# A three-stage attention and expert kernel: x parts in three joined pieces, and a rearranged hand-over

## The chip, the cores and the metric

The kernel runs on one core of a Trainium2 chip. The metric is the device time of one execution in microseconds, from the median of several runs. Engines: TensorE (PE, and PEld for its weight loads), VectorE (DVE), ScalarE (ACT), GpSimd (POOL), SyncE (SP), which issues the loads.

## The reference, cut to what matters

```
attn_out = attention(q, k, v)              # window 128 and 4 sink keys; 2 x 8 heads x 768 x 64
x = attn_out as 1536 rows of 512
assign each row to one of 8 experts, 192 rows each
for e in range(8):                          # w1[e] 512 x 1024, w2[e] 1024 x 512
    x[mask] = relu(x[mask] @ w1[e]) @ w2[e]
return ((x @ w_a) * (x @ w_b)) @ w_out      # 512 x 1536 twice, 1536 x 512
```

## The kernel before, in words

**Precision.** Every fp32 operand is kept as a high part, rounded to fp32r by a copy on ScalarE, and a low part, the difference, made on VectorE or GpSimd. A product is high x high, high x low and low x high.

**Experts.** After attention and routing, `expert(e)` runs eight times. An expert has four weight units u = 0 to 3 (two halves of w1, two of w2), each 128 x 2048. SyncE loads a unit to `raw[u]`, ScalarE rounds it in two halves (`split_hi`, L790), the low parts go to `ring_lo[u]`: for u = 0 to 2 on VectorE in halves (`split_lo`, L1012), for u = 3 on GpSimd in one instruction (L625). Each unit gives two groups g = 0, 1: ScalarE copies a part of the sum from PSUM (L936), VectorE adds (L1401 or L1404), and for u < 2 ScalarE and VectorE write the high and low part of h (L943, L1418). Unit u = 2, 3 of TensorE waits for `w_lo[u]`.

**Mixing stages.** The last product is done in two halves of the rows (c = 0, 1), each in six stages, so n = 0 to 11. Each half of 768 rows is two blocks of HT = 384. A stage has `mix(0, n)` (a factor of w_a), `down(n - 1)` (times w_out) and `mix(1, n)` (w_b). `mix` uses seven products P1, P6, P2, P7, P5, P4, P3 in that order instead of eight, with four sums of weight blocks (`add_blocks`, L688 to L695, GpSimd) and four sums T1 to T4 of blocks of x (`add_t`, L653 to L658, GpSimd). `round_mix(u, n, 0)` and `(u, n, 1)` on ScalarE round the plain blocks (L899, L900) and the sums (L904); `split_mix` on GpSimd makes the low parts (L704, four instructions, 1792 elements a partition); `round_out` (L913) and `split_out` (L718) do the same for w_out. `keep_p1` (L969) copies P1 from PSUM, and P2 on TensorE waits for it. `keep_a11` (L975) copies the first factor block. `round_g` (L982) and `lower_b` (L1433) split the product of the two factors for `down`.

**Parts of x.** The seven blocks of x of one half (B11, B21, B22, T1 to T4; 768 elements a partition each) are made in pieces of `PIECE` columns: `add_t(c, q)`, then `round_t(c, q)` (ScalarE, L923), then `split_t(c, q)` (GpSimd, L664). Before there are four pieces of 96 columns, with 7 instructions of 128 x 192 for each rounding and each low part. For c = 0 they stand in experts 4, 5, 6 and a fourth at the end of expert 6; for c = 1 the sums stand in stages n = 1 to 4, rounding and low parts in stages 2 to 5.

**What sets the order.** Each engine's list is written out by hand and runs in order; an instruction that waits for a semaphore holds up all behind it. In the last expert ScalarE's list has `round_mix(0,0,0)` after group (2,0), `round_mix(0,0,1)` after (2,1), `round_mix(1,0,0)` after (3,0), and `round_mix(1,0,1)` and `round_out(0)` behind the expert. GpSimd's list there is `split_lo(7, 3)` and then `add_blocks(0, 0)`, which waits for it, since the weight sums `s_sum` lie in `raw[3]`.

Of the kernel before, what the change touches and what calls it, by code (L numbers as in the profile page):

```python
# [5 lines left out]
def attention_moe_gated_product_kernel(  # L6
# [12 lines left out]
    f32 = mybir.dt.float32  # L19
# [37 lines left out]
    PIECE = HT // 4  # L57
# [16 lines left out]
    with ctx:  # L74
# [107 lines left out]
        t_tmp = sb("t_tmp", [P, 4, 2, PIECE])  # L182
# [211 lines left out]
        T4, T1, T2, T3, B11, B21, B22 = range(7)  # L394
# [17 lines left out]
        s_sum = raw[3][:, 0:4 * 2 * P].rearrange("p (b t m) -> p b t m", b=4, t=2)  # L412
        p1_sb = raw[2][:, 2 * DM:2 * DM + HT]
        u2_sb = raw[2][:, 2 * DM + HT:2 * DM + 2 * HT]
        u3_sb = raw[3][:, 4 * 2 * P:4 * 2 * P + HT]
# [16 lines left out]
        def t_block(c, b, low):  # L432

            if c == 0:
                return two(x_block(0, b) if low else t_first[:, b, :])
            if not low:
                return two(x_block(1, b))
            if b < 4:
                return two((ring[3], ring_lo[3])[b // 2][:, b % 2 * 2 * HT:(b % 2 + 1) * 2 * HT])
            return t_last[:] if b == B22 else two(x_block(b - B11, 7))  # L440

        def t_sources(c, q):

            first, second = (y[c][:, :, h * HT + q * PIECE:h * HT + (q + 1) * PIECE] for h in range(2))
            return {B11: first[:, 0:2, :], B21: first[:, 2:4, :], "B12": second[:, 0:2, :], B22: second[:, 2:4, :],
                    T4: t_tmp[:, T4], T1: t_tmp[:, T1], T2: t_tmp[:, T2], T3: t_tmp[:, T3]}

        def t_moves(c, q, low):

            qs = slice(q * PIECE, (q + 1) * PIECE)  # L450
            return [(b, t_block(c, b, low)[:, :, qs]) for b in (B11, B21, B22, T4, T1, T2, T3)]
# [114 lines left out]
        def _(pool):  # L566
# [78 lines left out]
            def add_t(c, q):  # L645

                src = t_sources(c, q)
                k = 4 * c + q
                if q == 0:
                    pool.wait_ge(grp_done, 8 * 4 * (c + 1))  # L650
                if k > 0:
                    pool.wait_ge(t_split, k)
                nc.gpsimd.tensor_tensor(src[T1], src["B12"], src[B11], ALU.subtract).then_inc(t_sums, 1)  # L653
                nc.gpsimd.tensor_tensor(src[T3], src[B22], src["B12"], ALU.subtract).then_inc(t_sums, 1)
                pool.wait_ge(t_sums, 4 * k + 1)
                nc.gpsimd.tensor_tensor(src[T2], src[B22], src[T1], ALU.subtract).then_inc(t_sums, 1)
                pool.wait_ge(t_sums, 4 * k + 3)
                nc.gpsimd.tensor_tensor(src[T4], src[B21], src[T2], ALU.subtract).then_inc(t_sums, 1)  # L658

            def split_t(c, q):  # L660
                src = t_sources(c, q)
                pool.wait_ge(t_rounded, 4 * c + q + 1)
                for (b, lo), (_, hi) in zip(t_moves(c, q, 1), t_moves(c, q, 0)):
                    op = nc.gpsimd.tensor_tensor(lo, src[b], hi.bitcast(f32), ALU.subtract)  # L664
                op.then_inc(t_split, 1)
# [3 lines left out]
            for e in range(4, E):  # L669
                if e < E - 1:  # L670
                    add_t(0, e - 4)
                split_lo(e, 3)
                if e < E - 1:
                    split_t(0, e - 4)
                if e == E - 2:
                    add_t(0, 3)
                    split_t(0, 3)
            def add_blocks(u, n):
# [5 lines left out]
                if k == 0:  # L684
                    pool.wait_ge(*expert_split(E - 1, 3))
                else:
                    pool.wait_ge(unit_lo[1 - u], n + u)
# [43 lines left out]
            for n in range(STAGES):  # L731
# [5 lines left out]
                if 2 <= n <= 5:  # L737
                    split_t(1, n - 2)
# [7 lines left out]
                if 1 <= n <= 4:  # L746
                    add_t(1, n - 1)
# [34 lines left out]
        def _(act):  # L782
# [132 lines left out]
            def round_t(c, q):  # L915

                src = t_sources(c, q)
                k = 4 * c + q
                if q == 0:
                    act.wait_ge(grp_done, 8 * 4 * (c + 1))  # L920
                act.wait_ge(t_sums, 4 * (k + 1))
                for b, dst in t_moves(c, q, 0):
                    op = nc.scalar.activation(dst, src[b], ACT.Copy)  # L923
                op.then_inc(t_rounded, 1)

            def expert(e, first):
                last = e == E - 1
                for u in range(4):
# [3 lines left out]
                    for g in range(2):  # L932
# [16 lines left out]
                        if e == E - 2 and (u, g) == (3, 1):  # L949
                            round_t(0, 3)  # L950
                        if last and (u, g) == (2, 0):
                            round_mix(0, 0, 0)
                        if last and (u, g) == (2, 1):
                            round_mix(0, 0, 1)
                        if last and (u, g) == (3, 0):
                            round_mix(1, 0, 0)
# [3 lines left out]
            round_mix(1, 0, 1)  # L960
            round_out(0)

# [21 lines left out]
            for n in range(STAGES):  # L984
# [7 lines left out]
                if 2 <= n <= 5:  # L992
# [15 lines left out]
        def _(dve):  # L1008
# [385 lines left out]
            def expert(e, first):  # L1394
                for u in range(4):
                    for s, bk in (EARLY_TILES[0] if u == 0 and first else late_tiles(e, u)):
                        split_x(s, bk)
                    for g in range(2):
# [21 lines left out]
                        if more and urgent:  # L1420
                            split_lo(e + 1, half // 2, half % 2)

# [33 lines left out]
            def factor_b(n):  # L1456
# [21 lines left out]
                lower_b(n, 1)  # L1478
                dve.wait_ge(products_b, 7 * n + P3)
# [3 lines left out]
                lower_b(n, 2)  # L1483
# [22 lines left out]
        def _(pe):  # L1506
# [301 lines left out]
            def mix(u, n):  # L1808
# [4 lines left out]
                if u == 0:  # L1813
                    if n % PAIRS_F == 0:
                        pe.wait_ge(t_split, 4 * (c + 1))
# [80 lines left out]
```

## Time and profile before

| what | us |
|---|---|
| median of 3 runs | 670.22 (668.29 to 672.74) |
| the profiled execution | 673.89 |
| its span | 672.1 |
| TensorE busy | 612.9 (91%) |
| VectorE / ScalarE / GpSimd busy | 402.1 / 320.4 / 329.8 |
| last experts' end, mixing stages | about 380; 382 to 666 |

The chain that ended last goes by TensorE for 68% of the span and by GpSimd for 16%. Matmul spans are modelled and overlap, so a stretch where TensorE is busy all the time is read against its neighbours, not as peak.

### The profile page before, as it was taken

The numbers are of one execution on the slowest core, as the hardware profiler recorded it, in microseconds if no ns is written. First come the engines' busy times: TensorE is split into PE (matmuls) and PEld (weight loads), VectorE is DVE, ScalarE is ACT, GpSimd is POOL, SyncE is SP. The second block draws the span as 40 slices with busy tenths as digits, with TensorE's granted clock in tenths as the row PEclk, the third lists the DMA queues.
The fourth block names the chain that finished last, engine by engine and source line by source line (L and its number), as shares of the span: only waits on it lengthen the run. The fifth ranks groups of instructions, "written<-read, shape, count | busy, mean of one in ns | idle before, by whom it ended". The sixth has DMA issues, their size and how long they took to land.

```text
span 672.1 us, 10960 instructions
## 1 busy us (share of the span) xinstructions
PE 612.9 (91%) x3840; PEld 548.3 (82%) x3840; DVE 402.1 (60%) x1060; ACT 320.4 (48%) x804; POOL 329.8 (49%) x371
## 2 busy tenths in 40 slices
PE   7999999999543999999997799999999999999995
PEld 4877766776322899999997799998999989999983
DVE  4567755764674377766874145665566466556654
ACT  3577656753231376767776333452453334344310
POOL 4000000000003321235787997999999888777623
PEclk8798999989655899999999889999999999999999
DMA  9974142130402456567565122221122242211002
GB/s 187 262 149 94 49 132 65 28 123 25 149 0 62 129 189 208 187 233 238 198 212 183 47 67 90 64 64 62 64 66 91 64 151 70 95 32 32 31 1 94
DMA packets 87512, 72.07 MB, mean 107 GB/s; under 512 B 39840, under 2 KB 74656, under 8 KB 87456
## 3 DMA queue, kind: packets, MB, share of 16 engines
q1 hardware_dynamic: 85536, 65.05, 33.1%
q0 software_dynamic: 1920, 6.29, 2.8%
q8 instruction: 32, 0.52, 0.3%
q14 instruction: 24, 0.20, 0.1%
HBM read 65.04 MB, written 6.29 MB: 106 GB/s over the span
## 4 chain that ended last, share of the span: by engine, by line
PE 68%; POOL 16%; DVE 7%; ACT 5%; issue 3%; DMA 1%; DVEq 0%; POOLq 0%; ACTq 0%
PE psum L1760 12%; PE psum L1838 6%; PE psum L1840 6%; PE psum L1841 6%; PE psum L1573 6%; PE psum L1761 6%; POOL w_lo L704 5%; PE psum L1753 3%; PE psum L1755 3%; PE psum L1754 3%; PE psum L1551 3%; PE psum L1538 3%; PE psum L1578 2%; PE psum L1515 2%; POOL x_hl L664 2%
## 5 line engine op out<-in xcount | busy, mean ns | idle before, releaser
L704 POOL TENSOR_TENSOR w_lo<-w_raw,w_hi 128x512 fp32r<-128x512 f32 x96 | 107.8, 1160 | 19.0 <-ACT w_hi L900 19.0
L1760 PE MATMUL psum<-h_hl,w_hi 128*128 128x384 f32 x256 | 77.3, 370 | 3.9 <-DVE h_hl L1418 3.8
L629 POOL MEMSET thr<- 128x8 f32 x1 | 0.1, 106 | 163.4 <-PE psum L1658 163.4
L1760 PE MATMUL psum<-x_hl,w_hi 128*128 128x384 f32 x256 | 76.8, 370 | 1.8 <-DVE x_hl L1387 1.6
L1840 PE MATMUL psum<-x_hl,w_hi 128*128 128x384 f32 x216 | 72.8, 337 | 0.0
L790 ACT ACTIVATE w_hi<-w_raw 128x1024 fp32r<-128x1024 f32 (+1 forms) x72 | 69.0, 958 | 0.0
L1494 DVE TENSOR_TENSOR o_acc<-psum,o_acc 128x512 f32<-128x512 f32 x60 | 41.5, 692 | 42.1 <-PE psum L1755 42.1
L1761 PE MATMUL psum<-x_hl,w_lo 128*128 128x192 f32 x256 | 65.0, 254 | 0.0
L1761 PE MATMUL psum<-h_hl,w_lo 128*128 128x192 f32 x256 | 65.0, 254 | 0.0
L1838 PE MATMUL psum<-t_first,w_hi 128*128 128x384 f32 x168 | 57.4, 341 | 6.4 <-ACT w_raw L969 4.1
L1753 PE MATMUL psum<-o_hi,g 128*128 128x512 f32 x144 | 56.1, 389 | 2.3 <-issue 2.3
L625 POOL TENSOR_TENSOR w_lo<-w_raw,w_hi 128x2048 fp32r<-128x2048 f32 x7 | 32.3, 4609 | 52.2 <-ACT w_hi L790 52.2
L1838 PE MATMUL psum<-x_hl,w_hi 128*128 128x384 f32 x168 | 56.3, 335 | 0.6 <-DVE w_raw L1447 0.6
L1841 PE MATMUL psum<-t_first,w_lo 128*128 128x384 f32 x168 | 56.7, 337 | 0.0
L1755 PE MATMUL psum<-o_hi,g 128*128 128x512 f32 x144 | 56.3, 391 | 0.0
L1754 PE MATMUL psum<-o_lo,g 128*128 128x512 f32 x144 | 56.2, 390 | 0.0
L1841 PE MATMUL psum<-x_hl,w_lo 128*128 128x384 f32 x168 | 56.2, 335 | 0.0
L1012 DVE TENSOR_TENSOR w_lo<-w_raw,w_hi 128x1024 fp32r<-128x1024 f32 x42 | 55.8, 1330 | 0.0
L904 ACT ACTIVATE w_hi<-w_raw 128x512 fp32r<-128x512 f32 x48 | 27.6, 624 | 53.6 <-POOL w_raw L695 53.6
L810 ACT ACTIVATE p_sb<-psum,nmax 128x264 f32<-128x264 f32 (+1 forms) x96 | 43.3, 459 | 20.3 <-DVE nmax L1038 20.3
L1760 PEld LDWEIGHTS psum<-h_hl,w_hi 128*128 128x128 f32 x256 | 49.0, 192 | 4.5 <-DVE w_lo L1012 3.3
L982 ACT ACTIVATE g<-psum 128x384 fp32r<-128x384 f32 x48 | 23.6, 492 | 60.9 <-DVE psum L1473 26.3
(220 smaller groups left out, 1606.3 us busy)
## 6 DMA issues: line engine op xcount, KB each, us to landing
w_raw<-in_moe_w_dram SPq DMA_DIRECT2D x32, 1024.0 KB, 5.5
w_raw<-in_moe_w_a_dram SPq DMA_DIRECT2D x12, 512.0 KB, 3.6
w_raw<-in_moe_w_b_dram SPq DMA_DIRECT2D x12, 512.0 KB, 3.5
w_raw<-in_moe_w_out_dram SPq DMA_DIRECT2D x12, 512.0 KB
k_raw<-in_k_dram SPq DMA_DIRECT2D x16, 192.0 KB, 3.8
q_raw<-in_q_dram SPq DMA_DIRECT2D x16, 192.0 KB, 4.1
v_sb<-in_v_dram SPq DMA_DIRECT2D x16, 192.0 KB, 4.2
xs_scratch<-x_rows SPq DMA_DIRECT2D x8, 384.0 KB, 3.4
```

Source lines behind the costliest of these rows:

```text
L704: return nc.gpsimd.tensor_tensor(out_t, t, hi_t.bitcast(f32), ALU.subtract)
L790: op = nc.scalar.activation(ring[slot][:, ps], raw[r][:, ps], ACT.Copy)
L810: op = nc.scalar.activation(p_sb[:, t % 2, h * SW:(h + 1) * SW][:, span(t, h)], bank[2 * (t % 2) + h][:, span(t, h)], ACT.Exp, scale=-1.0, ...
L1012: op = nc.vector.tensor_tensor(ring_lo[slot][:, hs], raw[slot][:, hs], ring[slot][:, hs].bitcast(f32), ALU.subtract)
L1753: nc.tensor.matmul(o, lhs_hi, rhs_hi, start=first, stop=False)
L1754: nc.tensor.matmul(o, lhs_hi, rhs_lo, start=False, stop=False)
L1755: return nc.tensor.matmul(o, lhs_lo, rhs_hi, start=False, stop=final)
L1760: nc.tensor.matmul(bk[:, 0:2 * CAP], lhs_hi, rhs_both, start=first, stop=False)
L1761: return nc.tensor.matmul(bk[:, 0:CAP], lhs_lo, rhs_hi, start=False, stop=final)
L1838: nc.tensor.matmul(o, w_h, t_hi[:, t, :], start=(first and t == 0), stop=False, skip_group_check=True)
L1840: nc.tensor.matmul(o, w_h, t_lo[:, t, :], start=False, stop=False, skip_group_check=True)
L1841: last = nc.tensor.matmul(o, w_l, t_hi[:, t, :], start=False, stop=(t == 1), skip_group_check=True)
```

## The change

The parts of x come in three pieces of 128 columns. Blocks that lie side by side are rounded and lowered together: 4 instructions of 512, 512, 512 and 256 elements a partition for a piece. T3 is written over the block B12 in y, so it waits for T1. The block order is changed to make this possible. Pieces of c = 0 stand in experts 4, 5 and 6; those of c = 1 have their sums in stages 1 to 3 and the rest in stages 2 to 4. `s_sum` moves to `raw[2]` beside the w_out unit, and the copies p1, u2, u3 to `raw[3]`. The last expert's unit 3 low parts are made by VectorE in two halves, after groups (1,1) and (2,0). ScalarE's first four `round_mix` come one group sooner, and `round_out(0)` comes after `keep_a11(0)`. In the last stage `lower_b` of part 2 comes before the P3 sum.

```diff
-    PIECE = HT // 4
+    PIECES = 3
+    PIECE = HT // PIECES
...
-        t_tmp = sb("t_tmp", [P, 4, 2, PIECE])
+        t_tmp = sb("t_tmp", [P, 3, 2, PIECE])
...
-        T4, T1, T2, T3, B11, B21, B22 = range(7)
+        T4, T1, T3, B22, B11, B21, T2 = range(7)
...
-        s_sum = raw[3][:, 0:4 * 2 * P].rearrange("p (b t m) -> p b t m", b=4, t=2)
-        p1_sb = raw[2][:, 2 * DM:2 * DM + HT]
-        u2_sb = raw[2][:, 2 * DM + HT:2 * DM + 2 * HT]
-        u3_sb = raw[3][:, 4 * 2 * P:4 * 2 * P + HT]
+        s_sum = raw[2][:, 2 * DM:2 * DM + 4 * 2 * P].rearrange("p (b t m) -> p b t m", b=4, t=2)
+        p1_sb, u2_sb, u3_sb = (raw[3][:, at * HT:(at + 1) * HT] for at in range(3))
...
-                    T4: t_tmp[:, T4], T1: t_tmp[:, T1], T2: t_tmp[:, T2], T3: t_tmp[:, T3]}
-
-        def t_moves(c, q, low):
-
-            qs = slice(q * PIECE, (q + 1) * PIECE)
-            return [(b, t_block(c, b, low)[:, :, qs]) for b in (B11, B21, B22, T4, T1, T2, T3)]
+                    T4: t_tmp[:, 0], T1: t_tmp[:, 1], T2: t_tmp[:, 2], T3: second[:, 0:2, :]}
+
+        def blocks_at(t, q):
+
+            return t.rearrange("p (m n) -> p m n", n=HT)[:, :, q * PIECE:(q + 1) * PIECE]
+
+        def t_moves(c, q):
+
+            first, second = (y[c][:, :, h * HT + q * PIECE:h * HT + (q + 1) * PIECE] for h in range(2))
+            x_c = x_hl[:, :, c * N:(c + 1) * N]
+            in_x = [blocks_at(x_c[:, t, :], q) for t in range(3)] + [blocks_at(x_c[:, 3, 0:2 * HT], q)]
+            sources = (t_tmp[:, 0:2].rearrange("p b t n -> p (b t) n"), second, first, t_tmp[:, 2])
+            if c == 0:
+                flat = t_first[:].rearrange("p b n -> p (b n)")
+                hi = [blocks_at(flat[:, t * 4 * HT:min((t + 1) * 4, 14) * HT], q) for t in range(4)]
+                return list(zip(hi, in_x, sources))
+            ends = x_hl[:, 3, :].rearrange("p (c z m n) -> p c z m n", c=2, z=2, n=HT)[:, :, 1, :,
+                                                                                       q * PIECE:(q + 1) * PIECE]
+            lo = [blocks_at(ring[3][:, 0:4 * HT], q), blocks_at(ring_lo[3][:, 0:4 * HT], q), ends,
+                  t_last[:, :, q * PIECE:(q + 1) * PIECE]]
+            moves = list(zip(in_x, lo, sources))
+            moves[2] = (*(t.rearrange("p (u m) n -> p u m n", u=2) if t is not ends else t for t in moves[2]),)
+            return moves
...
                 nc.gpsimd.tensor_tensor(src[T1], src["B12"], src[B11], ALU.subtract).then_inc(t_sums, 1)
+                pool.wait_ge(t_sums, 4 * k + 1)
                 nc.gpsimd.tensor_tensor(src[T3], src[B22], src["B12"], ALU.subtract).then_inc(t_sums, 1)
-                pool.wait_ge(t_sums, 4 * k + 1)
                 nc.gpsimd.tensor_tensor(src[T2], src[B22], src[T1], ALU.subtract).then_inc(t_sums, 1)
...
-            for e in range(4, E):
-                if e < E - 1:
-                    add_t(0, e - 4)
+            for e in range(4, E - 1):
+                add_t(0, e - 4)
                 split_lo(e, 3)
-                if e < E - 1:
-                    split_t(0, e - 4)
-                if e == E - 2:
-                    add_t(0, 3)
-                    split_t(0, 3)
+                split_t(0, e - 4)
...
                 if k == 0:
-                    pool.wait_ge(*expert_split(E - 1, 3))
+                    pool.wait_ge(*expert_split(E - 1, 2))
...
-                if 2 <= n <= 5:
+                if 2 <= n < 2 + PIECES:
                     split_t(1, n - 2)
...
-                if 1 <= n <= 4:
+                if 1 <= n < 1 + PIECES:
                     add_t(1, n - 1)
...
                         if 4 <= e < E - 1 and (u, g) == (2, 1):
                             round_t(0, e - 4)
-                        if e == E - 2 and (u, g) == (3, 1):
-                            round_t(0, 3)
+                        if last and (u, g) == (1, 1):
+                            round_mix(0, 0, 0)
                         if last and (u, g) == (2, 0):
-                            round_mix(0, 0, 0)
+                            round_mix(0, 0, 1)
                         if last and (u, g) == (2, 1):
-                            round_mix(0, 0, 1)
+                            round_mix(1, 0, 0)
                         if last and (u, g) == (3, 0):
-                            round_mix(1, 0, 0)
+                            round_mix(1, 0, 1)
 
             for e in range(E):
                 expert(e, e == 0)
-            round_mix(1, 0, 1)
-            round_out(0)
...
                 if n > 0:
                     round_mix(1, n, 1)
-                if 2 <= n <= 5:
+                else:
+                    round_out(0)
+                if 2 <= n < 2 + PIECES:
                     round_t(1, n - 2)
...
                             split_lo(e + 1, half // 2, half % 2)
+                        if e == E - 1 and (u, g) in ((1, 1), (2, 0)):
+                            split_lo(e, 3, u - 1)
...
                 lower_b(n, 1)
+                if n == STAGES - 1:
+                    lower_b(n, 2)
                 dve.wait_ge(products_b, 7 * n + P3)
...
-                lower_b(n, 2)
+                if n < STAGES - 1:
+                    lower_b(n, 2)
```

## Rows read from the trace of the kernel before

**Rows 1.** TensorE by windows: stretch, length, busy (x) of each engine, granted clock, DMA

```profile
365.00:370.00 5.00, 1.22 (x8) 0.99 (x8) 3.85 (x6) 4.08 (x8) 4.74 (x7) 1.00 0.24 79
387.80:390.60 2.80, 2.80 (x9) 2.80 (x10) 0.56 (x1) 0.49 (x1) 2.80 (x3) 0.50 0.01 3
```

**Rows 2.** TensorE's waits from 340 us on: total, times, longest

```profile
PE psum L1838 <- ACT w_raw L969: 4.1, 3, 3.2
```

**Rows 3.** ScalarE in order of time: start, duration, idle before and releaser in brackets

```profile
363.30 0.87 ACT L923 ACTIVATE t_first<-y 128x192 fp32r<-128x192 f32 x3 [5.64 <-POOL t_tmp L658]
...
385.26 1.15 ACT L904 ACTIVATE w_hi<-w_raw 128x512 fp32r<-128x512 f32 x2 [4.43 <-POOL w_raw L695]
386.31 1.04 ACT L913 ACTIVATE o_hi<-w_raw 128x1024 fp32r<-128x1024 f32 x1
387.26 0.47 ACT L969 ACTIVATE w_raw<-psum 128x384 f32<-128x384 f32 x1
```

**Rows 4.** GpSimd in order of time: low parts of unit (0,0)

```profile
377.71 4.45 POOL L704 TENSOR_TENSOR w_lo<-w_raw,w_hi 128x512 fp32r<-128x512 f32 x4
```

**Rows 5.** ScalarE: copies of group (2,0) in experts 5 and 6

```profile
332.01 0.33 ACT L936 ACTIVATE grp_sb<-psum 128x192 f32<-128x192 f32 x1 [1.50 <-PE psum L1761]
...
350.57 0.33 ACT L936 ACTIVATE grp_sb<-psum 128x192 f32<-128x192 f32 x1 [1.50 <-PE psum L1761]
```

**Rows 6.** GpSimd in experts 5 and 6: an x piece, one instruction of it, unit 3

```profile
317.75 2.70 POOL L664 TENSOR_TENSOR x_hl<-y,t_first 128x192 fp32r<-128x192 f32 x3 [6.85 <-ACT t_first L923]
318.86 1.59 POOL L664 TENSOR_TENSOR x_hl<-y,t_first 128x192 fp32r<-128x192 f32 x1
320.41 4.24 POOL L664 TENSOR_TENSOR x_hl<-t_tmp,t_first 128x192 fp32r<-128x192 f32 x4
...
345.64 4.63 POOL L625 TENSOR_TENSOR w_lo<-w_raw,w_hi 128x2048 fp32r<-128x2048 f32 x1
```

**Rows 7.** VectorE beside the blocked instruction

```profile
318.73 1.25 DVE L1012 TENSOR_TENSOR w_lo<-w_raw,w_hi 128x1024 fp32r<-128x1024 f32 x1
```

**Rows 8.** Three stages by windows, from down product to down product

```profile
431.76:454.54 22.78, 22.78 (x121) 21.34 (x121) 13.61 (x24) 10.24 (x23) 22.55 (x30) 1.00 0.23 70
454.54:477.74 23.20, 23.07 (x122) 21.31 (x121) 13.61 (x24) 10.10 (x23) 22.97 (x29) 1.00 0.21 69
477.74:501.27 23.53, 23.08 (x121) 21.32 (x121) 13.61 (x24) 10.15 (x24) 23.29 (x30) 1.00 0.22 68
```

**Rows 9.** GpSimd in these stages, in order of time

```profile
427.79 4.50 POOL L704 TENSOR_TENSOR w_lo<-w_raw,w_hi 128x512 fp32r<-128x512 f32 x4 [1.42 <-ACT w_hi L900]
...
438.36 0.73 POOL L695 TENSOR_TENSOR w_raw<-w_raw 128x256 f32<-128x256 f32 x1
...
461.84 0.74 POOL L695 TENSOR_TENSOR w_raw<-w_raw 128x256 f32<-128x256 f32 x1
...
469.47 0.61 POOL L653 TENSOR_TENSOR t_tmp<-y 128x192 f32<-128x192 f32 x1
...
471.84 0.74 POOL L688 TENSOR_TENSOR w_raw<-w_raw 128x256 f32<-128x256 f32 x1
...
474.76 4.51 POOL L704 TENSOR_TENSOR w_lo<-w_raw,w_hi 128x512 fp32r<-128x512 f32 x4
479.23 1.16 POOL L664 TENSOR_TENSOR x_hl<-y,x_hl 128x192 fp32r<-128x192 f32 x2
...
483.14 0.75 POOL L688 TENSOR_TENSOR w_raw<-w_raw 128x256 f32<-128x256 f32 x1
...
485.36 0.73 POOL L695 TENSOR_TENSOR w_raw<-w_raw 128x256 f32<-128x256 f32 x1
```

**Rows 10.** ScalarE in the last stage: part 2 of the factor product

```profile
655.47 0.49 ACT L982 ACTIVATE g<-psum 128x384 fp32r<-128x384 f32 x1 [0.57 <-DVE psum L1477]
```

**Rows 11.** VectorE in the last stage: low parts 2 and 3

```profile
656.88 1.21 DVE L1433 TENSOR_TENSOR g<-psum,g 128x384 fp32r<-128x384 f32 x2
```

More of the change, by code:

```diff
@@ L439, in t_block @@
                 return two((ring[3], ring_lo[3])[b // 2][:, b % 2 * 2 * HT:(b % 2 + 1) * 2 * HT])
-            return t_last[:] if b == B22 else two(x_block(b - B11, 7))
+            return t_last[:] if b == T2 else two(x_block(b - B11, 7))
         def t_sources(c, q):
@@ L647, in add_t @@
                 src = t_sources(c, q)
-                k = 4 * c + q
+                k = PIECES * c + q
                 if q == 0:
@@ L660, in split_t @@
             def split_t(c, q):
[L661 to L664, printed above, removed]
+                pool.wait_ge(t_rounded, PIECES * c + q + 1)
+                for hi, lo, src in t_moves(c, q):
+                    op = nc.gpsimd.tensor_tensor(lo, src, hi.bitcast(f32), ALU.subtract)
                 op.then_inc(t_split, 1)
@@ L915, in round_t @@
             def round_t(c, q):
-                src = t_sources(c, q)
-                k = 4 * c + q
+                k = PIECES * c + q
                 if q == 0:
@@ L921, in round_t @@
                 act.wait_ge(t_sums, 4 * (k + 1))
-                for b, dst in t_moves(c, q, 0):
-                    op = nc.scalar.activation(dst, src[b], ACT.Copy)
+                for hi, _, src in t_moves(c, q):
+                    op = nc.scalar.activation(hi, src, ACT.Copy)
                 op.then_inc(t_rounded, 1)
@@ L1814, in mix @@
                     if n % PAIRS_F == 0:
-                        pe.wait_ge(t_split, 4 * (c + 1))
+                        pe.wait_ge(t_split, PIECES * (c + 1))
                     if n == 0:
```

## The prediction, made before the change was run

> **What bounds the kernel now.** I read the stages by windows, then TensorE's waits, then the other engines in order of time. From the fourth w_out stage on, the mixing stages are TensorE's own: a plain one lasts 22.78 us and TensorE is busy for all of it, [rows 8], first line. The kernel loses time in two places, and both belong to the queues that feed TensorE.
>
> The first is the hand-over from the last expert to the first mixing unit. Of the 5 us after 365.0 TensorE works 1.22 [rows 1], and later it waits up to 3.2 us in one piece for ScalarE's L969 [rows 2]. Two causes stand in a row. ScalarE's second x round in expert 6 (fourth quarter) stood 5.64 us behind GpSimd's sums [rows 3], with expert 7's first group copy queued behind it. Then GpSimd's low parts of unit (0,0) ended at 377.71 + 4.45 = 382.16 [rows 4], its sums for unit (1,0) were ready for ScalarE at 385.26, and the kept P1 (L969), which TensorE's third product waits for, was queued behind that rounding and behind the w_out rounding: 387.26, so TensorE went on half a microsecond later, at 387.8, where the second window of [rows 1] begins (the sum takes 387.78). After these 3.2 us without work the granted clock was 0.50 for 2.80 us, the 1.2 GHz level: half of that, 1.40, is lost.
>
> The second is the mixing stages in which GpSimd also makes the parts of x for the second half. Call D the start of a stage's down product (the window's start) and L the start of L695, the last weight sum of unit (0, n+1). L - D is 6.60, 7.30 and 7.62 in the first three windows and these last 22.78, 23.20 and 23.53 [rows 8, 9]: a stage is long by L - D - 6.87 where that is positive. One more stage is like the third (+0.73), so the excess is 0.42 + 0.75 + 0.73 = 1.90 us. Between two L695 lie 23.5 us in which GpSimd never waits.
>
> **Hand-over.** The fourth quarter of x is gone from expert 6: no second x round, no second GpSimd turn. Expert 7 then follows in the rhythm of the group copies, 350.57 - 332.01 = 18.56 us [rows 5]: its group (2,0) is copied at 350.57 + 18.56 = 369.13.
> - Unit (0,0)'s first copy is now issued behind group (1,1), some 2 us ahead of this, and its sums are made by GpSimd right after the x piece, near 364, since GpSimd's own low parts of unit 3 (4.6 us, [rows 6]) are gone from in front of them; both are early. ScalarE's groups (2,0) to (3,1) get one rounding each queued ahead of them, and only the last, the (3,1) copy, is late by it (below). SyncE's loads of the first units and of w_out wait for the same low parts as before, which come earlier; they cost nothing. The roundings of the sums follow the (2,0) copy: 369.4 to 370.5 (1.15 for the two, [rows 3]).
> - VectorE makes both low halves of unit 3. The second comes after group (2,0): 369.85 to 371.1 (1.25, [rows 7]). TensorE could begin unit 3 some 0.5 behind the group, at 369.65, and waits until 371.3, then runs a quarter of the rhythm, 4.64, to 375.95. That stall of 1.6 is hidden by the chain below and too short for the clock, as far as these rows go.
> - A GpSimd instruction that starts inside such a VectorE instruction stands until it ends: one at 318.86 took 1.59 us where its three took 2.70 together, so the other two 0.56 each [rows 6, 7]. So GpSimd's third low part starts not at 370.6 but at 371.15, and the last two (2.5 of the 4.45, [rows 4]) end at 373.65.
> - From there as before: 382.16 to 385.26 is 3.10, the two roundings 1.05 (385.26 to 386.31), no w_out rounding (it moved behind the kept A11) but one group copy (0.33 long, [rows 5], of which some 0.1 overlaps, as 1.15 and 1.05 show), and 0.52 from L969 to TensorE [rows 3]. 373.65 + 3.10 + 1.05 + 0.25 + 0.52 = 378.57.
> - A product has 6 x 384 columns; a plain stage has 50,688 columns in 22.78 us [rows 8], so a product takes 1.04. TensorE has done two of unit (0,0) by 378.05 and idles 0.5.
>
> 387.78 - 378.57 = 9.21 gained, plus 1.40 of half clock that no long gap now causes. The w_out rounding then runs 380.05 to 381.1, GpSimd's w_out low parts 381.2 to 383.7, sums and low parts of unit (0,1) to 391.2, where TensorE wants them twelve products on, at 378.57 + 12.48 = 391.05; I charge 0.2. **Hand-over: -10.4 us.** Bounds: -12.8 if everything ran end to end from 365.04 (two expert units 9.28, two products 2.08: third product at 376.4, and 1.4 of clock); -3.8 if only the idle time of the first window went. Each step has its row, so I keep the computed value.
>
> The Trainium skill ("GPSIMD Engine Reference", section 8, Key points) says that GpSimd shares its SBUF interfaces with VectorE and contends with instructions that have two SBUF inputs. This speaks against moving the low parts to VectorE, which puts two such instructions beside GpSimd's low parts. If the whole of both (2 x 1.25) were lost to GpSimd instead of the 0.55 that I charge, the hand-over would give 8.4, the rival A below; the 1.59 us row agrees with the rule for starts inside, but a wide GpSimd instruction under two of them took 4.63 [rows 6], so an instruction already running is not held.
>
> **Joined pieces in the experts.** Per piece ScalarE and GpSimd have 4 instructions of 512, 512, 512 and 256 elements, as [rows 4]'s 4.45 us; before 7 of 192, 3.91 where nothing is in the way (479.23 to 483.14, [rows 9]) and 2.70 + 4.24 = 6.94 in expert 5, three starts blocked [rows 6]. Now also two or three starts are blocked: 4.45 + 2.1 = 6.5. The sums grow from 2.37 (469.47 to 471.84) to 3.05: four of 256, 2.92 (471.84 to 474.76), and one more wait for the one before, 0.13. So GpSimd is some 0.2 later with unit 3's low parts, which ended at 345.64 + 4.63 = 350.27 while TensorE needs them at about 351.1 (just behind the group of 350.57, [rows 5, 6]): covered, cost 0. Without that cover each 1 us later in experts 5 and 6 costs 1 us. ScalarE's share per piece is unchanged, 1.9. The exchange of s_sum and the p1, u2, u3 buffers costs nothing: it lets the sums start on unit 2's low parts.
>
> **Joined pieces in the mixing stages.** Here nothing hides them. A piece's low parts cost 4.45 + 0.02 = 4.47 against 3.91, its sums 3.05 against 2.37, in three stages instead of four. The first sums are absorbed: GpSimd stands 1.42 us for ScalarE behind them, before 427.79 [rows 9]. First stage: L - D = 6.60 + 0.56 = 7.16, excess 0.29. Second and third: GpSimd's 23.50 becomes 23.50 - 3.91 - 2.37 + 4.47 + 3.05 = 24.74, so each exceeds 22.78 by 1.96. The fourth: 23.50 - 6.28 = 17.2, none. Total 0.29 + 1.96 + 1.96 = 4.21 against 1.90: **+2.3 us**. The same work in fewer instructions, but packed into fewer stages that were already full. Bounds: if the joined ones cost no more than the old piece, 0; at 5.2 ns an element (6.94 over 1344), the slow rows of the experts, +16.8 (rival B). The mixing rows are much the nearer.
>
> **Tail.** In the last stage part 2's lowering moves ahead of the P3 sum and product. ScalarE rounds that part at 655.47 to 655.96 [rows 10]; VectorE lowered it at 656.88 [rows 11], now at 656.0, so the down product starts 0.88 sooner. The last part comes some 0.7 later, needed by tile 3 four us on: covered. **-0.9 us.** The bound above is 0, if something else holds the down product.
>
> **Sum:** -10.4 + 2.3 - 0.9 = -9.0. The profiled execution took 673.89 (span 672.1), giving 664.9; it stands 3.67 above the median of 670.22, so the timed median would be **661.2**.
>
> **The rivals.**
> - **A, the hand-over keeps a wait.** Contention on GpSimd (-8.4 there) or a TensorE gap on unit 3's low parts that reaches 3 us and halves the clock (another 1.4). For: four queues cross here. Against: the chain is short. Sum -7.0 to -5.6: 663.2 to 664.6. Chance 0.17.
> - **B, slower.** The joined instructions of the mixing stages run at the slow rows' rate: 9.3 us a piece. Excess is 3x - 9.2 for a piece of x us, so 18.7, or +16.8 on before: -10.4 + 16.8 - 0.9 = +5.5, 675.7. It decides from x = 7.5. Against: GpSimd's like-shaped four took 4.51 in these very stages [rows 9]. Chance 0.05.
> - **C, the pieces hold up the experts.** Each of experts 5 and 6 loses about 2 us, as GpSimd's low parts of unit 3 pass TensorE's need: 661.2 + 4.4 = 665.6. For: only 0.8 us of slack. Chance 0.12.
> - **D, the hand-over is all gained** and the mixing stages pay less: -12.8 + 1 - 0.9 = -12.7, 657.5. Chance 0.09.
> - That the rearrangement does nothing, since TensorE is bound anyway: the idle windows speak against it; 669 to 671, chance 0.05.
>
> **Numbers.** Forecast 0.52. A change of 1% is 6.7 us, about what a measurement can tell, so faster means below 663.5: forecast mostly (0.47), D, and part of A (0.06): 0.62. Within 1%: the rest of forecast and A, C and the last: 0.32. Slower by over 1%: 0.06, B and accidents. The range takes in D at one end and A and C at the other, 657.0 to 667.0.
>
> **What would show it.** Hand-over: no second x round in expert 6, the gap at 365 gone, third product of unit (0,0) near 378.6 at full clock, ScalarE's L969 behind a group copy and not behind the w_out rounding. Mixing: two stages of about 24.7 us and L695 about 8.8 after D, the next one plain. Experts: groups every 18.56 us. Tail: part 2 lowered before the P3 sum, the last down product 0.9 sooner after it. Wrong if the two long stages are near 30 us, if experts 5 and 6 lose time, or if TensorE idles over 3 us before the first product.

## The result, and the profile after

The changed kernel took 661.54 us (660.15 to 662.47), beside 670.22 (668.29 to 672.74) for the kernel before on the same chip: 8.7 less, a ratio of 0.987, 95% interval 0.982 to 0.991. These and all ratios below are of fast executions; a fourth one of the kernel before, 680.88, was in the chip's slower state and is left out. Its profiled execution took 662.47 (span 660.7), 11.4 less than the one of before.

I cut both traces at the same instructions. "Third product" is that of unit (0,0) which waits for the kept P1; D1 is the first down product. The second, third and fourth row make up the hand-over, from group (2,0) of expert 6 to D1. The forecast of the first row is its value before.

| stretch | before | predicted | after |
|---|---|---|---|
| to the (2,0) copy of expert 6 | 350.57 | 350.57 | 347.91 |
| (2,0) copy, expert 6 to expert 7 | 24.33 | 18.56 | 19.30 |
| from there to the third product | 12.88 | 9.44 | 9.57 |
| from there to D1 | 21.19 | 19.99 | 20.26 |
| D1 to D6 (where the pieces of c = 1 lie) | 115.81 | 118.12 | 118.08 |
| D6 to D12 | 132.75 | 131.87 | 131.00 |
| D12 to the end | 14.57 | 14.57 | 14.58 |

(D12 is the last down product.) The hand-over gave 9.27 of the 10.4 forecast. The 2.66 ahead of it and the 0.87 between D6 and D7 are not the change's: they are absent in a repeat of the same kernel (e5). Of the 2.66, 1.35 had been gained before the first expert product (218.32 in place of 219.67), in attention.

Two lines of the page after, busy times and the chain that ended last:

```profile
PE 606.7 (92%) x3840; PEld 541.9 (82%) x3840; DVE 410.2 (62%) x1062; ACT 317.0 (48%) x772; POOL 321.4 (49%) x330
...
PE 70%; POOL 14%; DVE 6%; ACT 5%; issue 3%; DMA 1%; DVEq 0%; ACTq 0%; POOLq 0%
```

TensorE's waits from 300 us on (total, times, longest), where [rows 2] had one of 3.2:

```profile
PE psum L1852 <- ACT w_raw L976: 3.5, 3, 1.7
PE psum L1774 <- DVE w_lo L1021: 1.8, 1, 1.8
PE psum L1767 <- issue: 1.4, 1, 1.4
PE psum L1774 <- POOL w_lo L641: 1.4, 2, 0.8
```

L976 is the kept P1: 0.23 us at the third product, the rest in the two long stages. L641 is unit 3's low parts on GpSimd, 0.85 and 0.51 us in experts 5 and 6, which I had forecast as covered. ScalarE in the last expert:

```profile
367.21 0.33 ACT L946 ACTIVATE grp_sb<-psum 128x192 f32<-128x192 f32 x1 [1.56 <-PE psum L1775]
...
374.97 1.16 ACT L915 ACTIVATE w_hi<-w_raw 128x512 fp32r<-128x512 f32 x2 [0.78 <-POOL w_raw L706]
376.03 0.32 ACT L946 ACTIVATE grp_sb<-psum 128x192 f32<-128x192 f32 x1
376.24 0.48 ACT L976 ACTIVATE w_raw<-psum 128x384 f32<-128x384 f32 x1
...
378.53 1.05 ACT L924 ACTIVATE o_hi<-w_raw 128x1024 fp32r<-128x1024 f32 x1
```

This is the order that was forecast: only a group copy stands between the rounding of the sums and L976, and the w_out rounding comes behind ([rows 3] had it in front). GpSimd beside it:

```profile
365.73 2.66 POOL L715 TENSOR_TENSOR w_lo<-w_raw,w_hi 128x512 fp32r<-128x512 f32 x2 [2.45 <-ACT w_hi L911]
368.66 3.19 POOL L715 TENSOR_TENSOR w_lo<-w_raw,w_hi 128x512 fp32r<-128x512 f32 x2 [0.28 <-ACT w_hi L915]
```

The second pair, beside VectorE's low half of unit 3, takes 3.19 against 2.66: the 0.5 charged for it is there. The five stages by windows, in the columns of [rows 8]:

```profile
397.04:419.82 22.78, 22.78 (x121) 21.34 (x121) 13.61 (x24) 10.28 (x20) 19.77 (x23) 1.00 0.23 70
419.82:442.89 23.07, 23.07 (x121) 21.30 (x121) 13.61 (x24) 9.42 (x19) 22.76 (x26) 1.00 0.21 69
442.89:467.64 24.75, 23.07 (x122) 21.30 (x122) 13.61 (x24) 10.14 (x21) 24.44 (x27) 1.00 0.20 65
467.64:492.33 24.69, 23.08 (x121) 21.31 (x121) 13.61 (x24) 8.90 (x18) 23.16 (x24) 1.00 0.19 64
492.33:515.12 22.79, 22.79 (x122) 21.35 (x122) 13.60 (x24) 8.41 (x16) 17.18 (x19) 1.00 0.21 70
```

Excess over 22.78 from the second on: 0.29, 1.97, 1.91 and nothing (forecast 0.29, 1.96, 1.96, 0). In the third GpSimd is busy for 24.44 of 24.75 and TensorE for 23.07. TensorE's own waits in the two long stages, 1.6 to 1.7 each, are for L976, which ScalarE reaches only after rounding GpSimd's sums. That GpSimd's load sets the length is tested by e1. Its last weight sums:

```profile
426.99 0.74 POOL L706 TENSOR_TENSOR w_raw<-w_raw 128x256 f32<-128x256 f32 x1
...
451.74 0.75 POOL L706 TENSOR_TENSOR w_raw<-w_raw 128x256 f32<-128x256 f32 x1
...
476.43 0.73 POOL L706 TENSOR_TENSOR w_raw<-w_raw 128x256 f32<-128x256 f32 x1
```

L - D is 7.17, 8.85 and 8.79 (forecast 7.16 for the first; 8.83 would follow from 1.96 + 6.87).

### The profile page after: what moved, and what is told of

It reads as the page before. It is cut to its first block, busy times and chain, and to the rows that moved or that the text cites. A ratio compares the mean times of both kernels' runs of the same rounds, so it can differ in the third digit from the quotient of the medians.

```text
span 660.7 us, 10889 instructions
## 1 busy us (share of the span) xinstructions
PE 606.7 (92%) x3840; PEld 541.9 (82%) x3840; DVE 410.2 (62%) x1062; ACT 317.0 (48%) x772; POOL 321.4 (49%) x330
## 4 chain that ended last, share of the span: by engine, by line
PE 70%; POOL 14%; DVE 6%; ACT 5%; issue 3%; DMA 1%; DVEq 0%; ACTq 0%; POOLq 0%
PE psum L1774 13%; PE psum L1852 6%; PE psum L1855 6%; PE psum L1854 6%; PE psum L1775 6%; PE psum L1587 6%; POOL w_lo L715 5%; PE psum L1767 4%; PE psum L1769 4%; PE psum L1768 4%; PE psum L1565 3%; PE psum L1552 3%; PE psum L1592 2%; PE psum L1529 2%; POOL x_hl L679 2%
## 5 line engine op out<-in xcount | busy, mean ns | idle before, releaser
L715 POOL TENSOR_TENSOR w_lo<-w_raw,w_hi 128x512 fp32r<-128x512 f32 x96 | 109.3, 1174 | 21.6 <-ACT w_hi L911 21.2
L1774 PE MATMUL psum<-h_hl,w_hi 128*128 128x384 f32 x256 | 75.4, 363 | 3.1 <-DVE w_lo L1021 1.8
L1774 PE MATMUL psum<-x_hl,w_hi 128*128 128x384 f32 x256 | 75.5, 366 | 1.6 <-DVE x_hl L1396 1.6
L1775 PE MATMUL psum<-x_hl,w_lo 128*128 128x192 f32 x256 | 64.8, 253 | 0.0
L1021 DVE TENSOR_TENSOR w_lo<-w_raw,w_hi 128x1024 fp32r<-128x1024 f32 x44 | 64.8, 1472 | 0.0
L1775 PE MATMUL psum<-h_hl,w_lo 128*128 128x192 f32 x256 | 64.2, 251 | 0.0
L641 POOL TENSOR_TENSOR w_lo<-w_raw,w_hi 128x2048 fp32r<-128x2048 f32 x6 | 27.7, 4610 | 50.7 <-ACT w_hi L801 50.7
L1774 PEld LDWEIGHTS psum<-h_hl,w_hi 128*128 128x128 f32 x256 | 48.0, 188 | 3.8 <-DVE w_lo L1021 2.0
```

The source lines that it names most:

```text
L715: return nc.gpsimd.tensor_tensor(out_t, t, hi_t.bitcast(f32), ALU.subtract)
L1021: op = nc.vector.tensor_tensor(ring_lo[slot][:, hs], raw[slot][:, hs], ring[slot][:, hs].bitcast(f32), ALU.subtract)
L1774: nc.tensor.matmul(bk[:, 0:2 * CAP], lhs_hi, rhs_both, start=first, stop=False)
L1775: return nc.tensor.matmul(bk[:, 0:CAP], lhs_lo, rhs_hi, start=False, stop=final)
```

## The experiments

Ratios are to the kernel before on the same chip, with 95% intervals. Unless it is said otherwise a kernel is the changed one with the edit shown, and nothing is left out of the computation. Where an edit is long, the fence tells it in words. The interval of every ratio overlaps that of the changed kernel (0.982 to 0.991; those of e1 and e11 only at its lower edge), so what a part is worth is read from the traces, not from the times. "Rhythm" is the distance between the same group copies of two experts, and "hand-over" is the sum of the three rows named above (before 58.40, changed 49.13). "Chain" is the distance from expert 7's (2,0) copy to the third product (changed: 9.57). "F to E" is from the first expert product to the end of the span (before 452.4, changed 442.4, the changed kernel again 446.6); it leaves out attention, which no kernel here touches.

**e1: the second half in four joined pieces.** It separates packing from the joining itself.

```diff
-    PIECES = 3
+    PIECES = (3, 4)          # by half; FIRST = (0, 3)
```

> The changed kernel, but the parts of x of the second half (c = 1) in four joined pieces of 96 columns, in stages 1 to 5 as before the change; the first half keeps three pieces. My theory (a mixing stage is long by L - D - 6.87, L the start of the last weight sum, D the start of the down product): a piece's low parts cost 3.5 us and its sums 2.45, so GpSimd's period falls from 24.7 to 23.2; L - D about 6.2, 6.6, 7.05, 7.3; excess 0, 0, 0.2, 0.4 instead of 0.3, 2.0, 1.9: 3.6 us faster than the changed kernel, near 658. Rival: what makes the two stages long is ScalarE's joined rounding or the new buffers, not GpSimd's load; then the excess stays about 4 us, only spread over more stages.

Ratio 0.978 (0.973 to 0.983). The stages:

```profile
422.29:445.08 22.79, 22.79 (x122) 21.34 (x121) 13.60 (x24) 9.97 (x20) 22.48 (x27) 1.00 0.21 70
445.08:467.87 22.79, 22.79 (x122) 21.35 (x122) 13.60 (x24) 9.99 (x20) 22.48 (x26) 1.00 0.23 71
467.87:490.72 22.85, 22.85 (x122) 21.30 (x121) 13.60 (x24) 9.84 (x20) 22.53 (x27) 1.00 0.21 70
490.72:513.90 23.18, 23.08 (x121) 21.32 (x121) 13.60 (x24) 8.23 (x16) 21.67 (x24) 1.00 0.21 69
```

The excess is 0.45 in place of 4.17 (and of 1.90 before). Joining is a gain; packing four pieces into three turned it into a loss. F to E is 442.6, 4.0 below the changed kernel in the same rhythm (e5), where 3.6 were expected. Against the changed kernel's first profile, 442.4, nothing shows, since that one had the shorter rhythm.

**e5: the changed kernel again.** Not an edit: it tells the change from the execution.

> The changed kernel once more, beside the others of this call. All theories: the stages as in its first trace (22.8, 23.1, 24.7, 24.7, 22.8); in the experts a rhythm of 18.56 us like the five others, not the 18.21 of its first trace, so 2 to 3 us above its first 661.5.

Ratio 0.987 (0.983 to 0.991), hand-over 49.29, stages 23.06, 24.70, 24.68 and again a plain one. But the expert rhythm was 18.56 as before, where the first profile of the same kernel had 18.21, and D6 to D7 was 23.72. The rhythm was expected; the median, 665.28 on another chip, is 3.7 above the first one's where 2 to 3 were. The hand-over is made up differently: 18.48 + 10.67 + 20.14. The chain is 1.1 longer because TensorE's 1.8 us wait was followed by half clock here:

```profile
371.00:374.00 3.00, 2.44 (x9) 2.44 (x10) 0.77 (x2) 0.65 (x2) 2.88 (x2) 0.63 0.00 0
374.00:377.00 3.00, 3.00 (x19) 3.00 (x19) 0.00 (x0) 0.00 (x0) 2.90 (x5) 0.80 0.58 174
```

and in the first profile of the same kernel it was not:

```profile
369.40:372.00 2.60, 2.48 (x17) 2.48 (x18) 0.33 (x2) 0.23 (x1) 2.46 (x3) 1.00 0.00 0
```

The number behind the five busy times is the granted clock: 0.63 and 0.80 against 1.00. In the matmuls of e5 one sees the 1.2 GHz level and its end:

```profile
371.56 0.53 PE L1774 MATMUL psum<-h_hl,w_hi 128*128 128x384 f32 x1 [1.79 <-DVE w_lo L1021]
...
374.72 0.57 PE L1774 MATMUL psum<-h_hl,w_hi 128*128 128x384 f32 x1
...
375.51 0.36 PE L1774 MATMUL psum<-h_hl,w_hi 128*128 128x384 f32 x1
```

Two products later the third starts at 379.91, with no wait for ScalarE left: TensorE had become the later of the two.

**e2: unit 3's low parts of the last expert on GpSimd again.**

```diff
+            split_lo(E - 1, 3)           # GpSimd, behind the experts' pieces
...
-                        if e == E - 1 and (u, g) in ((1, 1), (2, 0)):
-                            split_lo(e, 3, u - 1)
```

> The changed kernel, but the last expert's unit 3 low parts on GpSimd again, in one instruction ahead of the first weight sums. My theory: the instruction fits into GpSimd's idle time there (3.7 us before the first low parts of unit (0,0)), and VectorE no longer holds it up, so the third product of unit (0,0) starts within 0.7 us of the changed kernel's and the 1.8 us wait of TensorE for unit 3 goes; total within 1 us of the changed kernel. Rival: moving these low parts off GpSimd is what pays in the hand-over, and 3 to 4.6 us come back.

Ratio 0.987 (0.980 to 0.994), hand-over 49.21. The 1.8 us wait is gone, and the third product waits 2.48 instead (chain 10.05). The clock stays at 1.00 behind the 2.48. The chain lies between the changed kernel's 9.57 and its 10.67 with half clock (e5), so the move to VectorE gains 0.5 or loses 0.6: it trades one wait for another. In e2 the weight sums again wait for unit 3's low parts on GpSimd, so what the new place of `s_sum` gives the hand-over is undone here too.

**e3: ScalarE's order as before.**

```diff
-   round_mix after groups (1,1), (2,0), (2,1), (3,0); round_out after keep_a11(0)
+   round_mix after groups (2,0), (2,1), (3,0), behind the expert; then round_out(0)
```

> The changed kernel, but ScalarE's first four roundings of weights one group later, as before the change, and the w_out rounding and the second rounding of unit (1,0) ahead of the kept P1. My theory: the low parts of unit (0,0) end 1 us later and the kept P1 another 1 us later behind the w_out rounding, so 1.5 to 2 us slower than the changed kernel, with no half clock. Rival: the order carries most of the hand-over: 5 us or more come back, with a gap over 3 us and the half clock.

Ratio 0.990 (0.987 to 0.993), hand-over 51.43. The w_out rounding stands in front of the kept P1 (L977 here):

```profile
377.18 1.04 ACT L924 ACTIVATE o_hi<-w_raw 128x1024 fp32r<-128x1024 f32 x1
378.13 0.47 ACT L977 ACTIVATE w_raw<-psum 128x384 f32<-128x384 f32 x1
```

The third product waits 3.01, the chain is 11.82 (2.25 more), and then the clock falls:

```profile
378.65:382.00 3.35, 3.35 (x12) 3.35 (x13) 0.56 (x1) 0.49 (x1) 3.35 (x4) 0.58 0.08 20
```

From the third product to D1 it took 21.16, 0.9 more than with the changed order. The order is worth 2.25 + 0.9 against the changed kernel's first profile, and 1.15 + 1.0 against e5, which has the half clock itself; expected were 1.5 to 2 and no half clock.

**e4: the first half in four joined pieces, the fourth at the end of expert 6.**

```diff
-    PIECES = 3
+    PIECES = (4, 3)
...
+            add_t(0, 3)                  # GpSimd, behind the experts
+            split_t(0, 3)
...
+                        if e == E - 2 and (u, g) == (3, 1):
+                            round_t(0, 3)
```

> The changed kernel, but the parts of x of the first half in four joined pieces of 96 columns, the fourth at the end of expert 6 as before the change; the second half keeps three. My theory: ScalarE stands for GpSimd's sums at the end of expert 6 with expert 7's first group copy behind it, TensorE idles near 365, and 3 to 5 us of the hand-over gain are lost. Rival: the low parts moved to VectorE and the new order are what pays, and this costs under 1 us, since the joined quarter is short.

Ratio 0.994 (0.990 to 0.997), hand-over 52.72: 23.29 + 9.19 + 20.24. The step from expert 6 to 7 is long again, for the reason of [rows 3]:

```profile
361.95 0.53 ACT L939 ACTIVATE t_first<-t_tmp 128x384 fp32r<-128x384 f32 x1 [5.04 <-POOL t_tmp L678]
```

TensorE waits 2.04 and 0.70 us for it, and the 3.2 us behind them ran at a granted clock of 0.50. Pieces of 96 columns leave unit 3 of experts 5 and 6 without a wait: the rhythm into expert 6 is 18.56, where the changed kernel has 19.30.

**e6: unit 3's low parts ahead of the sums of x** in experts 4 to 6, against the 0.85 and 0.51.

```diff
             for e in range(4, E - 1):
-                add_t(0, e - 4)
                 split_lo(e, 3)
+                add_t(0, e - 4)
```

> The changed kernel, but GpSimd makes unit 3's low parts ahead of the sums of x in experts 4 to 6. My theory: TensorE's two waits for them (0.5 to 0.85 each, the rival C of the prediction in small) go, the sums still come in time for ScalarE's rounding, 1.3 us faster than the changed kernel. Rival: TensorE's time in the experts is set by VectorE, which the long GpSimd instructions hold up; then the waits only move to VectorE's low parts and nothing is gained.

Ratio 0.988 (0.985 to 0.991), hand-over 50.71. My theory fell. The waits for GpSimd are gone, but ScalarE now stands for the sums, its copies come late, and TensorE waits for h instead (the second row is a sum of two, the longer 0.7):

```profile
PE psum L1774 <- DVE w_lo L1021: 2.0, 1, 2.0
PE psum L1774 <- DVE h_hl L1427: 1.1, 2, 0.7
```

The steps between experts became 19.36 and 19.72, in an execution with the 18.21 rhythm; e7, with the same order in the other rhythm, has 18.56 and 19.26, together as much as e5's 19.31 and 18.48. Nothing is gained in either.

**e9: the first half's blocks one by one,** seven instructions of 256 elements a piece instead of four joined.

```diff
-                return list(zip(hi, in_x, sources))
+                return [each of the moves, cut into blocks of 2 x 128 columns]
```

> The changed kernel, but in experts 4 to 6 each joined copy and each joined low part is split into blocks of 256 elements (seven for a piece on each engine); the second half stays joined. My theory: the long GpSimd instructions hold VectorE's low parts of the weights (1.8 to 2.3 us instead of 1.2 to 1.6), and with short ones these go back under 1.7; but GpSimd itself is held at more starts, so the low parts of unit 3 come no earlier and TensorE's waits in experts 5 and 6 stay or grow to 1 us each: total equal to the changed kernel within 2 us. Rival: length is the harm, and with short ones both waits go, 1 us faster.

Ratio 0.989 (0.985 to 0.993). TensorE waits 1.5 and 0.8 for unit 3's low parts, the steps are 19.99 and 19.23, and the x piece takes 7.9 us against 7.4. VectorE is relieved (1.49 where the joined piece makes it 2.04; its three low parts beside the piece take 4.08 together, against 5.45 in the changed kernel and 4.25 before), while GpSimd takes longer:

```profile
315.36 1.49 DVE L1026 TENSOR_TENSOR w_lo<-w_raw,w_hi 128x1024 fp32r<-128x1024 f32 x1
```

**e10: the tail's order as before** (one execution).

```diff
-                if n == STAGES - 1:
-                    lower_b(n, 2)
```

> The changed kernel, but in the last stage part 2 is lowered behind the P3 sum and product, as before the change. My theory: the last down product starts 0.88 us later (its distance from the one before 17.95 us, not 17.07), the rest of the trace as before; the single time says nothing at this size. Rival: the last down product waits for something else, and its distance stays.

665.41 in one execution. The last down product comes 17.95 us after the one before, against 17.07; its wait is

```profile
PE psum L1764 <- issue: 2.3, 1, 2.3
```

against 1.4: 0.88, exactly the forecast term. The hand-over of this trace is 18.45 + 9.56 + 20.26.

**e7, e8, e11: combinations.** All have e1's pieces and the order of e11's first two edits below. e7 and e8 add e6's order, and e8 also e2's placement. e11 puts VectorE's halves of unit 3 sooner:

```diff
-                            round_mix(1, 0, 1)     # after group (3,0)
+   round_mix(1, 0, 1) behind keep_p1 of unit (0,0)
-   split_out(0) ahead of unit (0,1)'s low parts
+   split_out(0) behind them
-                        if e == E - 1 and (u, g) in ((1, 1), (2, 0)):
-                            split_lo(e, 3, u - 1)
+                        if e == E - 1 and u == 1:
+                            split_lo(e, 3, g)
```

> The changed kernel with the second half of x in four joined pieces, unit 3's low parts ahead of the sums in experts 4 to 6, unit (1,0)'s sums rounded behind the kept P1, and w_out's first low parts behind those of unit (0,1). My theory adds up: -3.6 (stages), -1.3 (experts), -0.5 to -2.5 (hand-over, since no chain by the kept P1 is left and TensorE's own work sets it): 5.5 to 7.5 us faster than the changed kernel of this call. Rival: the hand-over is bound by GpSimd's low parts whatever the order; then 4.9.

658.55 us, 0.981 (0.976 to 0.985); hand-over 48.26, F to E 441.1.

> As the one before, but the last expert's unit 3 low parts on GpSimd in one instruction. My theory: TensorE's 1.8 us wait for unit 3 goes, but GpSimd's low parts of unit (0,0) come 2 us later and set the first product; within 1 us of the one before. Rival: VectorE's part matters once the kept P1 no longer waits: 2 us slower.

660.83 us, 0.982 (0.980 to 0.984); hand-over 48.55, F to E 440.8. As the theory had it, the wait for unit 3 is gone and TensorE waits 1.19 for GpSimd's low parts of unit (0,0) instead. The median is 2.3 above e7's, as the rival had it, but F to E is 0.3 below e7's: the difference lies ahead of the experts and is not the edit's.

> The changed kernel with the second half in four joined pieces, unit (1,0)'s sums rounded behind the kept P1, w_out's first low parts behind those of unit (0,1), and VectorE's two halves of unit 3 in the last expert after groups (1,0) and (1,1) instead of (1,1) and (2,0); the order of the low parts in experts 4 to 6 as in the changed kernel. My theory: TensorE's wait of 1.8 to 2.0 us for unit 3, behind which the clock was at half in three of five traces, goes; 1 to 2 us faster than the best of the last call (658.5), near 657. Rival: GpSimd's low parts of unit (0,0), now under VectorE's, come later and TensorE waits for them instead: no gain.

659.51 us, 0.979 (0.975 to 0.983); hand-over 45.61 (18.50 + 7.03 + 20.08), F to E 439.0. TensorE has no wait between expert 7 and the stages:

```profile
368.00:371.00 3.00, 3.00 (x23) 2.97 (x22) 1.96 (x4) 2.33 (x7) 2.46 (x2) 1.00 0.00 0
371.00:374.00 3.00, 3.00 (x24) 3.00 (x23) 0.12 (x1) 0.86 (x3) 2.86 (x4) 1.00 0.00 0
```

F to E is the smallest of all, 7.6 below e5 in the same rhythm. In the timed runs the intervals of e1, e7 and e11 overlap, so that e11 is faster than e1 is shown by the traces alone; the 657 that was expected was missed. All three have central values of 0.981 or less (the changed one: 0.987, twice), but none is clear of the changed kernel's interval.

## Why the prediction was right

It was right in the mechanisms that carry the sum and nearly right in the sum; two of its claims failed, "covered, cost 0" and "too short for the clock". The terms are these.

**The sum.** The terms found give -9.27 + 2.27 - 0.88 = -7.9, and expert 5 loses 0.75 ahead of the hand-over (e5): -7.1 against a forecast of -9.0. The profiles give -11.4 (the first) and -7.5 (e5, span 664.6), the medians -8.7 and, on e5's chip, -8.4. From F to E they are -10.0 and only -5.8: the first has the shorter rhythm and lacks the 0.87 at D6 to D7, and e5 loses 1.1 in its first experts, before the first piece of x. The interval of e5's ratio (0.983 to 0.991, that is 6 to 12 us) holds all of these but the -5.8. So the forecast was somewhat too large by its own terms, and the timed runs can't tell the two apart. That the median came within 0.4 of the 661.2 forecast is in part luck.

**Hand-over, -10.4 forecast, -9.3 found.** Part by part: expert 6 to 7, -5.77 forecast and -5.03 found; the chain, -3.44 and -3.31; the third product to D1, -1.20 and -0.93. The working of the chain, 9.44, was right to 0.13: low parts slowed by 0.5, roundings, group copy, L976. The 5.77 holds more than the idle windows that the prediction names: in the kernel before there was a second stretch of half clock, in expert 7, from 370.30 to 373.54 at a granted clock of 0.50, behind waits of 3.06 and 0.72 us. It went with them. What failed is named next. By experiments: without the fourth quarter the step from expert 6 to 7 is 4.0 to 4.8 shorter (23.29 in e4, 18.45 to 19.30 without); ScalarE's order is worth 2.25 of the chain and 0.9 behind it (e3); the halves on VectorE next to nothing (e2). In e3 and e4 the total moves by less than the part (2.2 and 3.5), because what is undone in one part lets another run better: e4's chain is 9.19. The two were not undone together, so of the 9.2 some 3.5 is given to no part by an experiment.

**The failed step: "covered, cost 0"** for the pieces in the experts. I gave a piece 6.5 us and GpSimd a slack of 0.8. The piece takes 7.4, from 314.79 to 320.50 + 1.72 = 322.22:

```profile
314.79 1.29 POOL L679 TENSOR_TENSOR x_hl<-t_tmp,t_first 128x512 fp32r<-128x512 f32 x1 [6.29 <-ACT t_first L933]
316.04 4.50 POOL L679 TENSOR_TENSOR x_hl<-y,t_first 128x512 fp32r<-128x512 f32 x2
320.50 1.72 POOL L679 TENSOR_TENSOR x_hl<-t_tmp,t_first 128x256 fp32r<-128x256 f32 x1
325.34 4.59 POOL L641 TENSOR_TENSOR w_lo<-w_raw,w_hi 128x2048 fp32r<-128x2048 f32 x1
```

Unit 3's low parts end at 329.93, and TensorE goes on at 329.99 after 0.85 of waiting. From the (2,0) copy of the expert before they end 19.53 later, against 18.26 in the kernel before: GpSimd is 1.3 later, not 0.2, which is 0.5 more than the slack of 0.8. In the rhythm of 18.56 TensorE indeed waits 0.5 (e5), and in that of 18.21, which leaves less slack, 0.85.

Such a wait lengthens the step by 0.24 more than itself: 0.75 with a wait of 0.51 (e5, 18.56 to 19.31), 1.09 with 0.85 (first profile, 18.21 to 19.30). The first profile's second step is 19.30 too, but with a wait of only 0.51. The other 0.34 is TensorE's own. It starts a pair of products (L1774 and L1775) every 284.5 ns up to the wait, 62 pairs from 330.36 to 348.00, and every 290.0 ns behind it, 62 from 349.32 to 367.30, at a granted clock of 1.00. In e5 it goes the other way, 290.0 from 332.88 to 350.86 and 284.5 from 351.69 to 369.33, and this is why its second step is as short as 18.48. So the two steps came to 0.6 to 0.8 more than two plain ones (e1, e2, e3, e5, e10, e11) and to 2.2 more in the first profile, of which 1.84 is GpSimd's. It is rival C, at a seventh to a half of its 4.4. e4 (no wait with 96 columns) and e9 (more wait with more instructions) put the cause on the length of GpSimd's work for a piece. I counted blocked starts, and said that an instruction already running is not held. Beside that piece VectorE shows that holding goes the other way too:

```profile
317.35 2.04 DVE L1021 TENSOR_TENSOR w_lo<-w_raw,w_hi 128x1024 fp32r<-128x1024 f32 x1
```

That is 2.04 where [rows 7] had 1.25. It began inside a GpSimd instruction of 512 elements that ended near 318.3, and ended 1.1 behind that; the next GpSimd instruction, begun at 318.27, took 2.27 in turn, where one alone takes 1.25 to 1.31. The same at full size: VectorE's low half begun at 326.90, inside the 4.59 above, took 4.12 and ended at 331.02, 1.1 behind it. So the holding goes both ways: the one that starts inside the other's instruction stands until that ends, and the wider GpSimd's instructions, the longer VectorE stands. The Trainium skill ("GPSIMD Engine Reference", section 8, Key points) has this contention for VectorE instructions with two SBUF inputs; the trace agrees, 1.59 in [rows 6] and 2.04 here, and both engines pay.

**"Too short for the clock"** failed in some executions. The wait of 1.6 (1.76 to 1.97 measured) had half clock behind it in e1, e5 and e6, and full clock in the changed kernel's first profile, e7, e9 and e10. The granted clock of the 3 us behind it was 0.56, 0.53 and 0.57 in the ones, 1.00 in the others. In the changed kernel the chain was 10.67 with it (e5) and 9.57 and 9.56 without (first profile, e10): 1.1 us, near the 1.4 that rival A gave, though no gap of 3 us was needed. That the first profile, the one beside the forecast, ran without it was luck. The cover by GpSimd's chain was thin too: TensorE waited only 0.23 at the third product where I had it idle 0.5.

**Third product to D1:** 20.26 against 19.99. I charged 0.2 for the low parts of unit (0,1). The pause there is 0.34: starts 0.40 and 0.28 apart from 389.22 on, where the others are 0.17 apart; another 0.1 is lost at the third product's own start. With the w_out low parts behind that unit's, e7 has no pause and 19.76 (e11 a short one and 20.08).

**Mixing stages, +2.31 forecast, +2.27 found.** The relation held in each of the three stages with an excess: length = 22.78 + (L - D - 6.87) where that is positive. The sums of a piece took 3.03 (434.65 to 437.68; 3.05 forecast), its low parts 4.45 (445.06 to 449.51; 4.47). Rival B, the slow rate, had no part here: 4.45 is far from its 7.5. One reading ahead of the sum was off: the prediction has the stages as TensorE's own "from the fourth w_out stage on", but in the trace before, the plain ones (22.78 to 22.79) are the first two and those from D7 on.

**Tail, -0.9:** 0.88, by e10.

## What to carry to other kernels

When one engine feeds another in a fixed period, write down the lag at which the feeder starts to cost (here L - D of 6.87) and add up its work per period: fewer, wider instructions save only if the work is not also packed into fewer periods that are already full. A short stall is hidden only as long as the chain that hides it is longer by more than the stall's own side effects, half clock among them. Widening an elementwise instruction on GpSimd also lengthens what VectorE does beside it, so slack has to be counted on both engines. And a gain of this size has to be read from more than one trace of the same kernel: two of them differed here by 4.2 from F to E.

## What the runs showed of the hardware that was not expected

- The period of a plain expert was 18.20 to 18.21 us in some executions (changed, e6, e8, e9) and 18.56 in others (before, e1 to e5, e7, e10, e11); the changed kernel has shown both. Below it lie two distances between TensorE's pairs of products, 284.5 and 290.0 ns, both at a granted clock of 1.00. The distance stays for dozens of pairs and, in the traces here, changes only across a short gap of TensorE, in one and the same execution too (348.95 in the changed kernel, near 351 in e5). Which one follows a gap is open.
- Half clock followed waits of 1.78, 1.79 and 1.97 us in three executions and not waits of 1.76, 1.79, 1.80 and 1.97 in four others; the wait's length alone does not decide it. After 2.48 (e2) there was none either, and after 3.01 (e3) there was; so there was behind 2.04 and 0.70 in a row (e4) and behind 3.06 and 0.72 (before), and not behind the 2.23 at 382.21 (before).
- D6 to D7 took 23.66 to 23.85 in all traces but the changed kernel's first (22.78), most of it one wait of 0.6 to 0.8 for VectorE.
